# Pooling keys and values with VectorE's row sums instead of GpSimd's folds, in a fused attention and two-layer FFN kernel

## What is computed

```python
k_p = k.reshape(B, H, Sp, pool, D).mean(axis=3)      # pool = 8, Sp = 72
v_p = v.reshape(B, H, Sp, pool, D).mean(axis=3)
scores = scale * np.matmul(q, k_p.transpose(0, 1, 3, 2))
scores = scores - np.max(scores, axis=-1, keepdims=True)
attn = np.exp(scores)
attn = attn / (np.sum(attn, axis=-1, keepdims=True) + 1e-09)
attn_out = np.matmul(attn, v_p)                      # -> x, 4608 tokens x 512
h = x @ w_in;  g = np.maximum(0.01 * h, h);  x = g @ w_out
h = x @ w_in2; g = h * np.clip(h + 3.0, 0.0, 6.0) / 6.0; out = g @ w_out2
```

## Time and profile before

| | us |
|---|---|
| median of three runs | 1749.43 (1747.56 to 1751.18) |
| the profiled execution | 1742.31 |
| its span | 1740.5 |

### The profile page before, as it was taken

One profiled execution on the slowest core, in us unless ns is written; L12 is line 12 of the kernel. 1 busy time (PEld: TensorE's weight loads), 2 busy tenths in 40 slices (PEclk: granted clock), 3 DMA queues, 4 the chain that ended last, 5 costly groups with the idle time before them and its releaser, 6 DMA issues. The chain is left out here.

```text
span 1740.5 us, 34022 instructions
## 1 busy us (share of the span) xinstructions
PE 1692.8 (97%) x10794; PEld 1498.1 (86%) x10794; DVE 1037.1 (60%) x1851; ACT 641.8 (37%) x1305; POOL 552.3 (32%) x651
## 2 busy tenths in 40 slices
PE   7999999999999999999999999999999999999999
PEld 6787888888888888888999888989898888889898
DVE  8686767777686776766454654454544444544444
ACT  4554433433343333333232334343333333333332
POOL 6566674424334343322341303030302121121200
PEclk8899999999999999999999999999999999999999
DMA  5765677867677686767878767675757575767662
GB/s 146 229 197 173 209 243 239 262 208 252 206 232 237 202 260 191 244 202 233 283 214 287 257 178 219 176 222 176 219 177 220 176 221 171 223 174 223 173 200 78
DMA packets 218115, 366.85 MB, mean 211 GB/s; under 512 B 22464, under 2 KB 47040, under 8 KB 218048
## 3 DMA queue, kind: packets, MB, share of 16 engines
q1 hardware_dynamic: 218048, 366.04, 67.6%
HBM read 308.28 MB, written 57.67 MB: 210 GB/s over the span
## 5 line engine op out<-in xcount | busy, mean ns | idle before, releaser
L1412 PE MATMUL ps_h<-xs_hi,ring 128*128 128x256 f32 x3808 | 814.5, 282 | 19.8 <-ACT p L1052 5.5
L1412 PEld LDWEIGHTS ps_h<-xs_hi,ring 128*128 128x128 f32 x3808 | 638.6, 188 | 69.3 <-issue 27.6
L1412 PE MATMUL ps_h<-xs_lo,ring 128*128 128x256 f32 x1904 | 532.0, 279 | 0.0
L1412 PEld LDWEIGHTS ps_h<-xs_lo,ring 128*128 128x128 f32 x1904 | 357.9, 188 | 28.2
L949 ACT ACTIVATE g_hi<-gate 128x512 fp32r<-128x512 f32 x288 | 182.0, 632 | 425.9 <-DVE gate L1132 239.9
L1365 PE MATMUL ps_y<-g_hi,wout_hi 128*128 128x512 f32 x576 | 227.3, 395 | 0.3
L1367 PE MATMUL ps_y<-g_hi,wout_lo 128*128 128x512 f32 x576 | 227.1, 394 | 0.0
L1367 PE MATMUL ps_y<-wout_hi,g_lo 128*128 128x512 f32 x576 | 227.0, 394 | 0.0
L1365 PE MATMUL ps_y<-wout_hi,g_hi 128*128 128x512 f32 x576 | 226.1, 393 | 0.0
L1366 PE MATMUL ps_y<-g_lo,wout_hi 128*128 128x512 f32 x576 | 225.0, 391 | 0.0
L1366 PE MATMUL ps_y<-wout_lo,g_hi 128*128 128x512 f32 x576 | 224.8, 390 | 0.0
(11 more groups left out here) (128 smaller groups left out, 2335.4 us busy)
## 6 DMA issues: line engine op xcount, KB each, us to landing
ring<-w_in_split SPq DMA_DIRECT2D x920, 256.0 KB, 2.8
w_in_split<-ring SPq DMA_DIRECT2D x56, 256.0 KB, 3.9
w_in_split<-stage SPq DMA_DIRECT2D x56, 256.0 KB, 4.0
k_raw<-in_kT SPq DMA_DIRECT2D x32, 288.0 KB, 3.7
q_raw<-in_qT SPq DMA_DIRECT2D x32, 288.0 KB, 4.1
v_raw<-in_v SPq DMA_DIRECT2D x32, 288.0 KB
x0T<-x_stage SPq DMA_DIRECT2D x32, 288.0 KB, 3.9
x1T<-y_stage SPq DMA_DIRECT2D x36, 256.0 KB, 3.6
```

What stands on the lines that cost most here:

```text
L1412: mm = pe.matmul(banks[BANK_OF[r]], a, b[:, r, c, :], start=r in OPENS and c == 0 and n == 0, stop=c == 1 and n == 2, skip_group_check=True)
```

## The change

VectorE sums eight contiguous elements in one `tensor_reduce` for the keys and one for the values of a unit. For this the host lays out the keys as [KEYS, POOL] for each row and the values as [D, POOL]; the raw buffers have the same sizes, and the DMA of the values has one run of 4096 bytes for each of 72 partitions where it had two of 2048. ScalarE rounds `v_sum` into `v_hi` (`round_v`, two instructions of 72x64 for each unit); GpSimd keeps only `v_lo`. Units of batch elements 1 to 7 are done so (28 units). In batch element 0, GpSimd still folds keys of units 2 and 3 and all four units' values, now along the last axis with a stride of 8 elements, and VectorE's two key sums read contiguous data.

New places: VectorE sums keys at 10, 22, 34 and 52, values at 13, 25, 37 and 53, ScalarE rounds at 16, 28, 40 and 54 (unit 0 of the next batch element last, others first); tile 0 has its own lists, and unit 0 of batch element 1 is done at places 0, 2 and 3 of tile 0. `sum_v` on VectorE waits for the values' DMA and for `v_ready` of the unit before (GpSimd's `v_lo` has read `v_sum`); the wait on `pv_done` moves from GpSimd to ScalarE's `round_v`. In GpSimd's program `v_lo` stands where parts of the folds stood. VectorE's loop over tiles has one tile more written out behind it, because the last attention tile has no next unit 0.

```diff
@@ -58,6 +58,14 @@
 FIRST_LOAD_PLACES = (4, 18, 29, 40)
 FIRST_STORE_PLACES = (20, 31, 42, 52)
 FIRST_X_PLACES = (22, 33, 44, 54)
+
+
+SUM_K_PLACES = (52, 10, 22, 34)
+SUM_V_PLACES = (53, 13, 25, 37)
+ROUND_V_PLACES = (54, 16, 28, 40)
+FIRST_SUM_K_PLACES = (53, 13, 24, 35)
+FIRST_SUM_V_PLACES = (54, 16, 27, 38)
+FIRST_ROUND_V_PLACES = (55, 19, 30, 41)
 
 
 
@@ -149,8 +157,8 @@
             u = AttentionBuffers()
             if pad:
                 buf("pad", [P, pad // 4])
-            u.k_raw = buf("k_raw", [P, POOL, KEYS])
-            u.v_raw = buf("v_raw", [KEYS, 2, POOL * D])
+            u.k_raw = buf("k_raw", [P, KEYS, POOL])
+            u.v_raw = buf("v_raw", [KEYS, 2, D, POOL])
             u.q_raw = buf("q_raw", [P, 2, HALF])
             u.k_sum = buf("k_sum", [P, KEYS])
             u.v_sum = buf("v_sum", [KEYS, 2, D])
@@ -381,8 +389,7 @@
 
             def load_v(b, c):
                 above_zero(sp, v_summed, freed(b, c))
-                sp.dma_start(buffers(b, c).v_raw[:], v[b, 2 * c:2 * c + 2].rearrange(
-                    "h (k e) d -> k h (e d)", e=POOL)).then_inc(v_loaded[c], 16)
+                sp.dma_start(buffers(b, c).v_raw[:], v[b, c]).then_inc(v_loaded[c], 16)
 
             def load_unit(b, c):
                 load_k_q(b, c)
@@ -646,47 +653,45 @@
 
         @block.gpsimd
         def _(pool):
-            def sum_k(b, c, folds):
-
-                u, raw_k = buffers(b, c), buffers(b, c).k_raw
-                pool.wait_ge(k_loaded[c], 16 * (b + 1))
-                for i, rows in enumerate((POOL // 2, POOL // 4)):
-                    nc.gpsimd.tensor_tensor(raw_k[:, 0:rows], raw_k[:, 0:rows],
-                                            raw_k[:, rows:2 * rows], ALU.add
+            def sum_k(c, folds):
+
+                u, raw_k = buffers(0, c), buffers(0, c).k_raw
+                pool.wait_ge(k_loaded[c], 16)
+                for i, width in enumerate((POOL // 2, POOL // 4)):
+                    nc.gpsimd.tensor_tensor(raw_k[:, :, 0:width], raw_k[:, :, 0:width],
+                                            raw_k[:, :, width:2 * width], ALU.add
                                             ).then_inc(folded, 1)
                     pool.wait_ge(folded, folds + i + 1)
-                above_zero(pool, qk_ready, 3 * freed(b, c))
-                nc.gpsimd.tensor_tensor(u.k_sum[:], raw_k[:, 0], raw_k[:, 1], ALU.add
+                nc.gpsimd.tensor_tensor(u.k_sum[:], raw_k[:, :, 0], raw_k[:, :, 1], ALU.add
                                         ).then_inc(k_summed, 1)
 
-            def sum_v(b, c, folds):
-
-                u, n, raw_v = buffers(b, c), 4 * b + c, buffers(b, c).v_raw
-                pool.wait_ge(v_loaded[c], 16 * (b + 1))
-                for i, width in enumerate((POOL * D // 2, POOL * D // 4)):
-                    nc.gpsimd.tensor_tensor(raw_v[:, :, 0:width], raw_v[:, :, 0:width],
-                                            raw_v[:, :, width:2 * width], ALU.add
+            def sum_v(c, folds):
+
+                u, raw_v = buffers(0, c), buffers(0, c).v_raw
+                pool.wait_ge(v_loaded[c], 16)
+                for i, width in enumerate((POOL // 2, POOL // 4)):
+                    nc.gpsimd.tensor_tensor(raw_v[:, :, :, 0:width], raw_v[:, :, :, 0:width],
+                                            raw_v[:, :, :, width:2 * width], ALU.add
                                             ).then_inc(folded, 1)
                     pool.wait_ge(folded, folds + i + 1)
-                above_zero(pool, pv_done, 2 * freed(b, c))
                 for hd in range(2):
                     nc.gpsimd.tensor_tensor(u.v_hi[:, hd, hd * D:(hd + 1) * D],
-                                            raw_v[:, hd, 0:D], raw_v[:, hd, D:2 * D], ALU.add
+                                            raw_v[:, hd, :, 0], raw_v[:, hd, :, 1], ALU.add
                                             ).then_inc(v_hi_ready, 1)
-                nc.gpsimd.tensor_tensor(u.v_sum[:], raw_v[:, :, 0:D], raw_v[:, :, D:2 * D],
+                nc.gpsimd.tensor_tensor(u.v_sum[:], raw_v[:, :, :, 0], raw_v[:, :, :, 1],
                                         ALU.add).then_inc(v_summed, 1)
+                pool.wait_ge(v_summed, c + 1)
+                v_lo(0, c)
+
+            def v_lo(b, c):
+
+                u, n = buffers(b, c), 4 * b + c
                 pool.wait_ge(v_hi_ready, 2 * n + 2)
-                pool.wait_ge(v_summed, n + 1)
                 for hd in range(2):
                     nc.gpsimd.tensor_tensor(
                         u.v_lo[:, hd, hd * D:(hd + 1) * D], u.v_sum[:, hd, :],
                         u.v_hi[:, hd, hd * D:(hd + 1) * D].bitcast(F32), ALU.subtract
                     ).then_inc(v_ready, 1)
-
-            def sum_unit(b, c):
-                folds = 4 * (PAIRS * b + c) - 4
-                sum_k(b, c, folds)
-                sum_v(b, c, folds + 2)
 
             def blocks_lo(i):
 
@@ -779,70 +784,47 @@
                 pool.memset(u.v_lo[:].bitcast(F32), 0.0).then_inc(v_zeroed, 1)
             pool.wait_ge(v_zeroed, 2 * PAIRS)
             pool.sem_inc(k_summed, 2)
-            sum_k(0, 2, 0)
-            sum_v(0, 0, 2)
-            sum_k(0, 3, 4)
-            sum_v(0, 1, 6)
-            sum_v(0, 2, 8)
-            sum_v(0, 3, 10)
+            sum_k(2, 0)
+            sum_v(0, 2)
+            sum_k(3, 4)
+            sum_v(1, 6)
+            sum_v(2, 8)
+            sum_v(3, 10)
             blocks_lo(0)
             blocks_lo(1)
-            sum_unit(1, 0)
-            sum_k(1, 1, 16)
+            v_lo(1, 0)
             blocks_lo(2)
             blocks_lo(3)
-            sum_v(1, 1, 18)
-            sum_k(1, 2, 20)
+            v_lo(1, 1)
...
@@ -993,9 +975,22 @@
                     nc.scalar.activation(u.x0_stage[:, half, :], u.ps[:, half, 0:HALF],
                                          ACT.Copy, scale=V_SCALE).then_inc(x0_copied, 1)
 
-            def attention_at(T, place):
+            def round_v(b, c):
+                u, n = buffers(b, c), 4 * b + c
+                act.wait_ge(v_summed, n + 1)
+                act.wait_ge(pv_done, 2 * freed(b, c))
+                for hd in range(2):
+                    nc.scalar.activation(u.v_hi[:, hd, hd * D:(hd + 1) * D], u.v_sum[:, hd, :],
+                                         ACT.Copy).then_inc(v_hi_ready, 1)
+
+            def attention_at(T, place, next_unit=True):
                 for name, c in stages_at(T, place):
                     stage(name, T + 1, c)
+                if is_first(T) and place == 3:
+                    round_v(1, 0)
+                for c, at in enumerate(FIRST_ROUND_V_PLACES if is_first(T) else ROUND_V_PLACES):
+                    if place == at and (c > 0 or next_unit):
+                        round_v(T + 1 if c else T + 2, c)
 
             def next_x(T, i, m, places):
                 if i == HF - 1:
...
@@ -1202,9 +1199,8 @@
                 u, n = buffers(b, c), 4 * b + c
                 if name == "sum_k":
                     dve.wait_ge(k_loaded[c], 16)
-                    nc.vector.tensor_reduce(
-                        u.k_sum[:], u.k_raw[:].rearrange("p e k -> p k e"),
-                        AXIS_X, ALU.add).then_inc(first_k_summed, 1)
+                    nc.vector.tensor_reduce(u.k_sum[:], u.k_raw[:], AXIS_X, ALU.add
+                                            ).then_inc(first_k_summed, 1)
                 if name == "split_x":
                     dve.wait_ge(first_x_hi, c + 1)
                     nc.vector.tensor_tensor(xp_lo[:, c], first_chunk(c),
@@ -1254,7 +1250,28 @@
                                             u.pT_hi[:].bitcast(F32), ALU.subtract
                                             ).then_inc(pT_ready, 1)
 
-            def attention_at(T, place):
+            def sum_k(b, c):
+                dve.wait_ge(k_loaded[c], 16 * (b + 1))
+                dve.wait_ge(qk_ready, 3 * freed(b, c))
+                nc.vector.tensor_reduce(buffers(b, c).k_sum[:], buffers(b, c).k_raw[:], AXIS_X,
+                                        ALU.add).then_inc(k_summed, 1)
+
+            def sum_v(b, c):
+                dve.wait_ge(v_loaded[c], 16 * (b + 1))
+                dve.wait_ge(v_ready, 2 * freed(b, c))
+                nc.vector.tensor_reduce(buffers(b, c).v_sum[:], buffers(b, c).v_raw[:], AXIS_X,
+                                        ALU.add).then_inc(v_summed, 1)
+
+            def attention_at(T, place, next_unit=True):
+                if is_first(T) and place == 0:
+                    sum_k(1, 0)
+                if is_first(T) and place == 2:
+                    sum_v(1, 0)
+                for c in range(0 if next_unit else 1, PAIRS):
+                    if place == (FIRST_SUM_K_PLACES if is_first(T) else SUM_K_PLACES)[c]:
+                        sum_k(T + 1 if c else T + 2, c)
+                    if place == (FIRST_SUM_V_PLACES if is_first(T) else SUM_V_PLACES)[c]:
+                        sum_v(T + 1 if c else T + 2, c)
```

(6 more changed lines are left out.)

67 lines of the change are left out of this document (25 added, 42 removed).

## The result

The kernel after takes 1733.76 us (median of four runs, 1732.85 to 1735.43) against 1750.31 us for the kernel before, timed beside it (median of four runs, 1747.56 to 1751.19; three of them are those of the table). The ratio is 0.9911 with a 95% interval of 0.9898 to 0.9923: 16.5 us faster, where 10.5 were forecast. The profiled execution's own time is 1735.43 us.

A forecast was written before the change was run, and what follows sets the result against it. TensorE, busy 97% of the span, was taken as the bound, so GpSimd's relief counts only where TensorE waits. Gains of 7.5 (tile 1), 2.6 (tiles 2 to 6) and 0.4 (opening), 10.5 us, gave 1738.9 us; range 1729 to 1752.

The forecast's parts named there:

- the low ends taken: VectorE's new row sums: 0.75 us for keys and 1.2 for values, against high ends of 1.19 and 2.12 us.
- Tile 1, 7.5 us forecast: Tile 1: 8.1 us gained from shorter TensorE waits, 0.6 taken back by ScalarE's roundings at places 16 and 40.
- The chain through SP: Tile 1: values' load waiting for GpSimd's sum delays the store, then ScalarE's copy; TensorE's 1.15 and 2.27 us waits go.
- `ring`, 1.8 us: Tile 1: TensorE's wait for `ring` goes, since folds of two sums stand right ahead of `t_sums` and `sums_lo`.
- `u` and `pT_lo`: Tile 1: half of the 3.7 us left of TensorE's waits for these VectorE results is gained, 1.85 us.
- Tiles 2 to 6, 2.6 us forecast: Tiles 2 to 6 together: 5.5 us gained from shorter waits, less 2.9 lost to ScalarE's roundings.
- The copy's waits: Tiles 2 to 6: TensorE waits 3.7 us, 13 times, for ScalarE's copy at L1057; 1.7 us of it follows lengthened `gate`s.
- the forecast 5.5 us of gain: Tiles 2 to 6: 1.7 us of copy waits, 1.65 of `pT_lo` waits, 2.2 from 0.17 us at some 13 waits.
- the 2.9 us of loss: Tiles 2 to 6: ScalarE's roundings ahead of the copy cost 0.57 us a tile, 0.11 in step 2 and 0.46 in step 5.
- 0.46 were forecast: Step 5 of tiles 2 to 6: roundings of 0.51 us ahead of the copy, 0.05 spare, delay part 4 by 0.46 us.
- Opening and tile 0: Opening gains 0.4 us by a shorter key sum, tile 0 nothing; GpSimd's strided folds may lose up to 6.8 us.
- The base: 10.5 us, reckoned on an execution of 1742.31 us, were subtracted from the three-run median of 1749.43, 7.1 us above it.

The follow-up runs named there:

- e11_values_summed_twice: The kernel after, with VectorE summing each unit's values twice, first into a spare tile; 1747.51 us, ratio 0.9989 to the kernel before.
- e1_before_again: The kernel before, unchanged, timed and profiled a second time; 1748.6 us, ratio 1.0007, span of the profile 1746.6 us.
- e2_after_again: The kernel after, unchanged, timed and profiled a second time; 1734.54 us, ratio 0.9927 to the kernel before, span 1729.9 us.
- e5_store_ahead: The kernel before, with the stores of units 0 to 2 one place earlier in tiles 1 to 6, ahead of the loads; 1745.92 us, ratio 0.9997.
- e9_weights_ahead: The kernel before, with SP loading tile 1's step 3 raw weights ahead of the unit's keys and values; 1744.34 us, ratio 0.9978.
- e8_round_later: The kernel after, with ScalarE's roundings at places 17, 29, 41 instead of 16, 28, 40; 1733.45 us, ratio 0.9921 to the kernel before.
- e10_weights_ahead_folds_behind: As e9_weights_ahead, on the kernel before, with GpSimd's `sum_v(2, 0)` also moved behind `t_sums(1)` and `sums_lo(0)`; 1744.94 us, ratio 0.9977.
- e4_no_folds: The kernel before without GpSimd's two halvings of keys and values, summing only two of eight rows; 1727.54 us, ratio 0.9882.
- e7_dummy_folds: The kernel after, with twelve unread 128x128 additions on GpSimd ahead of each `v_lo` in batch elements 1 to 7; 1745.12 us, ratio 0.9985.

## Why the prediction came out right, and where its steps did not

**Row sums.** 0.75 and 1.2 us, the low ends taken, against 740 and 1204 ns. The two key sums of the opening decide what no row of before told apart: the same 576 elements into 72 results take 754 ns contiguous and 1190 strided, so the price was the stride's. A price of the number of results doesn't show: 0.14 us and 1.04 ns an element fit all three sums, 588 ns for 432 elements into 6 results, 740 for 576 into 72 and 1204 for 1024 into 128. The Trainium skill's rule of 16-byte lines (SBUF — State Buffer, Door 1: The DMA port swizzle) agrees with these two numbers. The Trainium skill's advice to consider restructuring a `tensor_reduce` on a hot path (VectorE: DVE Perf Modes, Rules for kernel authors) spoke against this change, and the measurement decides against it here: the kernel is 16.5 us faster with the sums, and by e11_values_summed_twice most of that is gone at twice the length of the values' sum.

**Tile 1, 7.5 us forecast.** Measured 6.3 between the first two profiles and 9.8 between e1_before_again and e2_after_again. The place and the engine were right, the steps were not all:
- The chain through SP: right that the load of values holds SP (22.7 to 5.1 us, no wait over 3 us, as said), wrong in what is behind it. The step that failed is the one that reads the 2.27 us as the store's. e5_store_ahead takes the store out: the 1.15 us for `x_stage` go, with no gain in time, and the wait for `pT_lo` stays (3.8 us there). e9_weights_ahead moves the weights' load and the wait for `pT_lo` falls to 1.15 us. I had read the row that ended ScalarE's 4.38 us and stopped; the wait for `pT_lo` five us later had a wait of ScalarE's for `s_sum` of its own ahead of it (1.80 us, until 230.53).
- `ring`, 1.8 us, was to go and fell to 1.1. The wait at the start of the tile went; a new one came in step 7, since `v_lo` waits for ScalarE's rounding with `sums_lo` behind it. The prediction had asked what stands behind `round_v` on ScalarE, and not what stands behind `v_lo` on GpSimd, where the wait was added.
- `u` and `pT_lo`: of 3.7 us left I took half, 1.85. `u` alone fell by 1.9. The reason given, that `gate` is shorter without the folds, doesn't hold in tile 1, where its mean grew (932 ns after, 867 and 788 before); what made `u` come sooner is open.
- The wait of 2.12 us at the tile's end (GpSimd's sums of x behind its folds, then `xs_lo`, then VectorE's `h`, a chain that no run takes apart) was not read. It fell to 0.40, and with it went the fall of the clock behind it in e1_before_again. It makes up for waits that grew, for ScalarE's `h` from 0.6 to 1.7.

**Tiles 2 to 6, 2.6 us forecast.** Measured 3.2 and 6.5 us in the two pairs of profiles, an estimated 1.5 of the 6.5 being the lowered clock behind tile 1's end. `gate` and `prob` did get shorter. The copy's waits fell in number (13 to 7) and little in time (3.7 to 3.4, in e2_after_again 2.7 us), those for `pT_lo` did not (3.3 to 3.6), so most of the forecast 5.5 us of gain did not come out of these two waits. Less than half of the 2.9 us of loss came: this is the mis-sized term. I took two roundings of 255 ns as 0.51 us. They are 241 ns each, but back to back they overlap, and what they take of ScalarE's time is 0.30 us, 447.75 to 448.05:

```profile
447.75 0.39 ACT L983 ACTIVATE v_hi<-v_sum 72x64 fp32r<-72x64 f32 x2
448.05 0.36 ACT L1053 ACTIVATE h<-ps_h 128x256 f32<-128x256 f32 x1
...
448.07 0.40 PE L1386 MATMUL ps_y<-g_hi,wout_lo 128*128 128x512 f32 x1
448.55 0.36 PE L1431 MATMUL ps_h<-xs_hi,ring 128*128 128x256 f32 x1
```

Part 4 starts 0.48 us after the matmul before it; 0.23 is normal, so 0.25 us are lost in this tile where 0.46 were forecast, and e8_round_later, with the roundings out of the way, gains nothing that shows. The Trainium skill (ScalarE: Activation LUTs, What ACT_TABLE_LOAD costs) has back-to-back ACTIVATEs overlap by about 93 ns; here a pair of 241 ns is shown with 0.39 us, which agrees.

**Opening and tile 0.** Forecast 0.4 us of gain and up to 6.8 of loss. The key sums did get shorter (2 x 0.44 us), and the two stretches are 2.5 us longer from the first profile of before to that of after and 0.3 us from e1_before_again to e2_after_again: no gain, and no loss outside the spread. GpSimd's strided folds are not the longer ones (below).

**The base.** The forecast took a sum of 10.5 us from the median, reckoned on an execution 7.1 us below it. That execution had shorter waits in tile 1 than e1_before_again, and its clock did not fall behind them. So most of the gain that e9_weights_ahead isolates can't be seen in it: tile 1 of e9_weights_ahead is 1.4 us shorter than that of the first profile and 4.2 us shorter than that of the second. From the first profile of before to that of after the gain is 6.8 us, less than the forecast; between the second ones it is 16.7, more. The forecast lies between the two by terms of which some did not come as reasoned and others were not in it, and how near its number came is in part luck.

What stays open: after e9_weights_ahead some 5 us of tile 1 are left between it and the kernel after. e10_weights_ahead_folds_behind tried one of their places and gained nothing; the sums of x at the end of the tile (2.14 us still in e9_weights_ahead) and the waits for `u` (3.0 us) were not tried one by one. That GpSimd's time makes them, directly or through the queues behind it, is shown in sum by e4_no_folds; e7_dummy_folds shows only that such time can cost as much, in other waits. How much of the gain in tiles 2 to 6 is due to the shorter instructions of VectorE no run shows, since e7_dummy_folds left them short.

## What to carry to other kernels

Follow a wait back past the first releaser and note, for each queue on the way, everything that stands behind the waiting instruction: here the load in front held up not its neighbour in the listing but four weight loads, three engines away from TensorE. Moving work to the engine with the fuller load can pay if its instructions fit about into the idle stretches where they stand; the engine that is relieved matters for what is queued on it, not for its busy share. Before taking a profiled execution as the base of a sum, compare its own time with the runs: one 0.4% below the median may lack the very stall that the change removes, and one 0.5% above it, as that of e5_store_ahead, has more than the usual ones.
